# Attention with a mixer on one Trainium2 core: the products with v over 64 columns of TensorE

## The reference, cut to what matters

```python
B, H, S, D = 4, 8, 576, 64
q_rot, k_rot = rotate(q), rotate(k)                       # rotary embedding
scores = q_rot @ k_rot.T / sqrt(D)
attn = exp(scores - max(scores)); attn /= sum(attn) + 1e-9
x = (attn @ v) laid out as [B, S, H * D]
h = max(x.T @ w_tok1, 0) @ w_tok2                         # mixer
u = x + h.T
out = u + max(u @ w_ch1, 0) @ w_ch2
```

## Time and profile before

| | |
|---|---|
| median of 3 runs | 677.58 us (674.8 to 677.66) |
| the profiled execution, its own time | 677.07 us |
| its span, first to last instruction | 675.2 us |
| PE busy in the span | 650.1 us (96%) |
| DVE, ACT, POOL busy in the span | 449.6, 390.2, 296.1 us |
| first V of tile 4, first pair to last pair | 29.67 to 319.92 us |

### The profile page before, as it was taken

How to read it: one execution, slowest core, us unless ns; L and a number is a source line. 1 busy time by engine, 2 the same in 40 slices (tenths; PEclk the granted TensorE clock), 3 DMA queues, 4 the chain that set the end, 5 groups by cost and what they waited for, 6 DMA issues and landing times.

```text
span 675.2 us, 19627 instructions
## 1 busy us (share of the span) xinstructions
PE 650.1 (96%) x7796; PEld 627.6 (93%) x7796; DVE 449.6 (67%) x844; ACT 390.2 (58%) x725; POOL 296.1 (44%) x276
## 2 busy tenths in 40 slices
PE   3999999999999999999999999999999999999997
PEld 2999999999999999999899999999999999999997
DVE  5576766666766666666545598548974489644895
ACT  3455556565555565665547355677646775476753
POOL 4656567766665566522570000484004840048300
PEclk9999999999999999999999999999999999999999
DMA  4234433344433544311600233100031000310002
GB/s 131 73 99 116 130 87 107 101 109 112 116 108 104 149 111 134 87 53 34 205 2 1 63 126 102 48 1 2 2 102 47 0 0 2 99 48 1 1 2 71
DMA packets 52177, 48.73 MB, mean 72 GB/s; under 512 B 15104, under 2 KB 44352, under 8 KB 52096
## 3 DMA queue, kind: packets, MB, share of 16 engines
q1 hardware_dynamic: 51792, 47.52, 24.8%
q10 hardware_dynamic: 304, 0.07, 0.0%
HBM read 30.77 MB, written 9.44 MB: 60 GB/s over the span
## 4 chain that ended last, share of the span: by engine, by line
PE 96%; ACT 1%; DVE 1%; issue 0%; DVEq 0%
PE rest L648 24%; PE slot L604 10%; PE slot L1158 8%; PE slot L1160 8%; PE slot L1159 8%; PE rest L543 7%; PE rest L1158 6%; PE rest L1160 6%; PE rest L1159 6%; PE slot L600 3%; PE slot L1190 2%; PE rest L1190 2%; PE slot L543 1%; PE rest L224 1%; PE rest L221 1%; ACT pt L762 1%
## 5 line engine op out<-in xcount | busy, mean ns | idle before, releaser
L648 PE MATMUL rest<-v,pt 64*128 64x65 f32 x2304 | 152.5, 272 | 7.8 <-ACT pt L762 7.1
L648 PEld LDWEIGHTS rest<-v,pt 64*128 64x128 f32 x2304 | 147.0, 189 | 10.9 <-ACT pt L762 9.4
L840 DVE TENSOR_REDUCE neg_max<-slot 128x1 f32<-128x576 f32 x144 | 108.6, 756 | 71.1 <-PE slot L604 67.8
L1149 POOL TENSOR_TENSOR w_ch_part<-w_ch_sums,w_ch_part 128x512 fp32r<-128x512 f32 x21 | 31.0, 1475 | 178.0 <-ACT w_ch_part L1400 178.0
L762 ACT ACTIVATE pt<-rest 128x320 f32<-128x320 f32 x128 | 55.6, 435 | 88.6 <-PE rest L543 88.6
L1464 ACT ACTIVATE pieces<-h 128x288 fp32r<-128x288 f32 x168 | 73.8, 444 | 49.9 <-PE slot L1160 26.4
L604 PE MATMUL slot<-turned_k,turned_q 64*128 64x288 f32 x256 | 88.2, 436 | 2.3 <-ACT moved_q L776 1.6
L604 PE MATMUL slot<-moved_k,moved_q 64*128 64x288 f32 x256 | 88.2, 436 | 0.0
L1555 DVE TENSOR_TENSOR pieces<-h,pieces 128x288 fp32r<-128x288 f32 x168 | 74.3, 452 | 9.3 <-ACT pieces L1464 8.8
L851 DVE COPY pt<-rest 128x320 f32<-128x320 f32 x128 | 61.7, 482 | 14.8 <-PE rest L543 14.8
L751 ACT ACTIVATE prob_a<-slot,neg_max 128x576 f32<-128x576 f32 x80 | 59.2, 740 | 15.9 <-DVE neg_max L840 12.8
(11 more groups left out here) (248 smaller groups left out, 1922.8 us busy)
## 6 DMA issues: line engine op xcount, KB each, us to landing
moved_q<-turned_q SPq DMA_DIRECT2D x31, 160.0 KB, 2.5
raw_qk<-in_q_dram SPq DMA_DIRECT2D x16, 256.0 KB, 2.6
raw_v<-in_v_dram SPq DMA_DIRECT2D x16, 256.0 KB, 2.7
x_scratch<-x_pair SPq DMA_DIRECT2D x16, 256.0 KB, 2.0
stage_or_x<-x_scratch SPq DMA_DIRECT2D x16, 256.0 KB, 4.0
raw_qk<-in_k_dram SPq DMA_DIRECT2D x15, 256.0 KB, 2.9
w_ch_whole<-in_moe_w_ch_dram SPq DMA_DIRECT2D x8, 384.0 KB, 3.5
w_ch_A_whole<-in_moe_w_ch_dram SPq DMA_DIRECT2D x4, 768.0 KB, 7.8
```

What stands on the lines that cost most here:

```text
L648: return pe.matmul(rest[:, 2 + r, at:at + V], x[rows, j, :], w[rows, j, :], start=begins, stop=ends, skip_group_check=True)
L840: dve.tensor_reduce(neg_max[p % 2][:, i:i + 1], score_slot(p, i)[:, :, 0:HALF], AX.XY, ALU.max, negate=True).then_inc(maxed, 1)
```

## The change

The diff is cut to its core. What it does:

- V no longer splits the 128 rows of the array but its 128 columns. One product contracts all 128 keys of a chunk and has only 64 query columns as weights (`cols`); its output is 64 partitions. The two query halves of a tile are two such products, one for columns 0 to 63 and one for 64 to 127. A tile has 10 products in every case (the tail chunk takes keys 448 to 575, and the rows of `v` that would count twice are zero). Tile 4 takes v of head A for its upper queries and v of head B for its lower ones, so `pt_both` and its zeros go.
- The sum of a head is complete in one bank: head A in bank 2, head B in bank 3. `sum_o` and `y` are gone. `guard` reads the bank, and `normalise` moves from POOL to DVE and reads the bank too.
- V calls stand in groups, (5, 6), (7, 8), (0), (1, 2), (3, 4), and score calls too. There are 7 `pt` buffers in place of 5 and the two `pt_both`.
- The first V of a head waits for that head's `normalise` of the pair before (`x_done`) in place of `o_summed`.
- On SP `store(p - 1)` stands behind `move("k", 0, p + 1)`. The v tail is one transfer and no longer two.

```diff
-    TURNED = 5
+    TURNED = 7
-    RAW = {"k": 2 * 16, "q": 3 * 16, "v": 3 * 16}
+    RAW = {"k": 2 * 16, "q": 3 * 16, "v": 2 * 16}
...
+    def output(h):
+
+        t0, t1 = HEADS[h]
+        return rest[:, 2 + "AB".index(h), 0:(t1 - t0) * V].rearrange("p (t d) -> p t d", d=V)
...
-            store(p - 1)
             if not no(p + 1):
                 sp.wait_ge(scores, p * TILES + G + 1)
             move("k", 0, p + 1)
+            store(p - 1)
             move("q", 0, p + 1)
...
         def values(p, i):
...
-            elif i == 0:
-                pe.wait_ge(o_summed["B"], p)
             if i == 0:
                 pe.wait_ge(v_copied, 2 * p + 1)
             if i == G:
-                pe.wait_ge(o_summed["A"], p + 1)
                 pe.wait_ge(v_copied, 2 * p + 2)
...
+            if p > 0 and i in (0, G):
+                pe.wait_ge(x_done, 2 * (p - 1) + a + 1)
+            to = output("AB"[a])[:, i - HEADS["AB"[a]][0], :]
+            for j in range(NG):
+                for r, cols in enumerate((top, low)):
+                    w = v_sb[r if i == G else a][:, j, :]
+                    mm = pe.matmul(to[cols], pt_of(p, i)[:, j, cols], w, start=(j == 0), stop=(j == G), skip_group_check=True)
             mm.then_inc(o_added, 1)
...
-        def sum_o(p, h):
-            if no(p):
-                return
-            t0, t1 = HEADS[h]
-            dve.wait_ge(o_added, p * TILES + t1)
-            if p > 0:
-                dve.wait_ge(x_done, 2 * (p - 1) + "AB".index(h) + 1)
-            dve.tensor_reduce(y[h][:].rearrange("p t d -> p (t d)"), rest[:, 2:4, 0:(t1 - t0) * V].rearrange("p r n -> p n r"),
-                              AX.X, ALU.add).then_inc(o_summed[h], 1)
...
+        def normalise(p, h):
+            if no(p):
+                return
+            a, (t0, t1) = "AB".index(h), HEADS[h]
+            dve.wait_ge(inv_done, 2 * p + a + 1)
+            if p > 0:
+                dve.wait_ge(x_stored, p * STORED)
+            dve.tensor_tensor(x_pair[:, 1 - a:NG, a, :], output(h)[:, :, 0:D],
+                              inverse[p % 2][:, t0:t1].unsqueeze(2).broadcast_to([P, t1 - t0, D]), ALU.mult).then_inc(x_done, 1)
```

More of the change, by code:

```diff
@@ L536, in gpsimd @@
                 w1.split_lo(pool, p - (N - 2))
-        normalise(N - 1, "B")
     def tensor(pe):
@@ L617, in turn @@
             pe.wait_ge(exped, g + 1)
[L618 to L619 removed]
             for j in range(NG):
+                at = j * P if j < G else S - P
                 for r, rows in enumerate((top, low)):
[L622 to L624 removed]
+                    mm = half_turn(rest[:, r, j * D:(j + 1) * D], prob[i][rows, at:at + P], r)
             mm.then_inc(turned, 1)
@@ L678, in tensor @@
             score(p, 0)
+            score(p, 1)
             turn(p - 1, 7)
+            values(p - 1, 5)
             values(p - 1, 6)
-            score(p, 1)
             turn(p - 1, 8)
+            score(p, 2)
+            score(p, 3)
+            turn(p, 0)
             values(p - 1, 7)
-            score(p, 2)
-            turn(p, 0)
             values(p - 1, 8)
+            turn(p, 1)
             transposes("k", p + 1)
-            turn(p, 1)
+            score(p, 4)
+            turn(p, 2)
             values(p, 0)
-            score(p, 3)
-            turn(p, 2)
-            score(p, 4)
+            score(p, 5)
+            turn(p, 3)
+            score(p, 6)
             values(p, 1)
-            turn(p, 3)
-            score(p, 5)
             values(p, 2)
@@ L698, in tensor @@
             turn(p, 4)
+            score(p, 7)
+            score(p, 8)
+            turn(p, 5)
             values(p, 3)
-            score(p, 6)
-            score(p, 7)
-            turn(p, 5)
             values(p, 4)
-            score(p, 8)
             turn(p, 6)
-            values(p, 5)
         first, p = slot[0], N
         turn(p - 1, 7)
+        values(p - 1, 5)
         values(p - 1, 6)
@@ L729, in slot_left @@
         elif k == 3:
-            pe.wait_ge(o_summed["B"], N)
+            pe.wait_ge(x_done, 2 * N)
     def scalar(act, h1_of_batch_0):
@@ L757, in copy_up @@
                 return
-            to, before = pt_both[0] if i == G else pt_of(p, i), last_on_pt(p, i)
             act.wait_ge(turned, p * TILES + i + 1)
-            if before is not None and before >= 0:
-                act.wait_ge(o_added, before + 1)
-            act.activation(to[:, :, top], rest[:, 0, 0:NG * D].rearrange("p (j n) -> p j n", j=NG), ACT.Copy).then_inc(up_done, 1)
+            pt_free(act, p, i)
+            act.activation(pt_of(p, i)[:, :, top], rest[:, 0, 0:NG * D].rearrange("p (j n) -> p j n", j=NG), ACT.Copy).then_inc(up_done, 1)
         def weights_hi(n):
@@ L778, in scalar @@
         for p in range(N):
-            copy_up(p - 1, 7)
             exponent(p, 0)
+            exponent(p, 1)
             copy_up(p - 1, 8)
@@ L846, in copy_low, with guard @@
                 return
-            to, before = pt_both[1] if i == G else pt_of(p, i), last_on_pt(p, i)
             dve.wait_ge(turned, p * TILES + i + 1)
-            if before is not None and before >= 0:
-                dve.wait_ge(o_added, before + 1)
-            dve.tensor_copy(to[:, :, low], rest[:, 1, 0:NG * D].rearrange("p (j n) -> p j n", j=NG)).then_inc(low_done, 1)
-        def sum_o(p, h):
+            pt_free(dve, p, i)
+            dve.tensor_copy(pt_of(p, i)[:, :, low], rest[:, 1, 0:NG * D].rearrange("p (j n) -> p j n", j=NG)).then_inc(low_done, 1)
+        def guard(p, h):
             if no(p):
@@ L922, in vector @@
         token.split_lo(dve, 0, 3)
-        sum_o(p - 1, "B")
+        guard(p - 1, "B")
+        invert(p - 1, "B")
         token.split_lo(dve, 0, 4)
-        guard(p - 1, "B")
+        normalise(p - 1, "B")
         w1.split_lo(dve, 2)
-        invert(p - 1, "B")
     def last_store(sp):
```

142 lines of the change are left out of this document (46 added, 96 removed).

## The result

| | before | after |
|---|---|---|
| median of 4 runs | 677.48 us (674.8 to 677.66) | 644.73 us (641.5 to 646.36) |
| ratio | | 0.952, 95% interval 0.948 to 0.956 |
| profiled execution, its span | 675.2 us | 639.5 us (time 641.5) |
| TensorE's mean granted clock | 1.00 | 0.997 |

The changed kernel is 4.8% faster, 32.8 us by the medians. 638 us was predicted, with 612 to 664 as the range.

What follows compares the result with a forecast made beforehand. PE bounds the kernel. Per pair 19.36 - 4.5 (V) + 1.5 (switches) - 0.5 - 0.1 (waits, scores) = 15.7 us, 16.8 with the q move; 15 pairs save 38.4 us, last tiles 0.6: 638 us; range 612 to 664.

Steps and rivals of the forecast that it cites:

- The bound: PE's own work sets the pace; V is bound by loading 128 columns of weights, 56 ns an instruction, not by streaming.
- The price of V: V's 180 instructions a pair, loading 64 columns, fall from 56 to 31 ns each: 4.5 us less per pair.
- Rival 3: Column tiles do not load side by side; V stays at 56 ns an instruction, 691 us; chance 0.14.
- rival 4: Load and product of V take turns, about 108 ns an instruction, near 840 us; chance 0.04.
- The switches: PE going to column tiling for V and back costs 0.3 us a group, 1.5 us a pair; bounds 0.75 to 2.0.
- The removed wait and the other engines: PE's wait for `sum_o` goes, 0.5 us a pair; `x_done` costs nothing; DVE, POOL and ACT add nothing.
- rival 2: Small waits of PE for copies, maxima and exponents add 0.5 to 1.5 us a pair, 645 to 661 us; chance 0.16.
- One sign: Sign that the forecast is right: DVE's idle time ahead of the maxima shrinks to a third.
- The move of q: `moved_q`, behind three stores on SP, lands at 16.3 to 17.3 us; PE idles about 1.1 us once a pair.
- Rival 1: The move of q is hidden: 15.7 or 15.0 us a pair, 622 to 611 us; chance 0.11.

Runs made afterwards that it cites:

- Experiment 6: Also `before_33`: the kernel before, with V streaming 33 columns of v in place of 65, half of v left out; 687.52 us, ratio 1.016.
- experiment 8: The kernel before, with V loading only 64 of its 128 query columns, row halves kept, lower 64 queries of each tile left out; 639.91 us, ratio 0.946.
- store_split: Experiment 2: the changed kernel with only the two small tail stores on SP moved behind the move of q; 622.97 us, ratio 0.922.
- experiment 3: Also `nine_groups`: `store_last` with every V call between two turns or scores of its own, nine groups a pair in place of five; 655.33 us, ratio 0.968.
- experiment 4: `store_last` with one tiny product in row halves between the two V calls of three groups; 642.84 us, ratio 0.950.
- store_last: Experiment 1: the changed kernel with all of store(p - 1) on SP moved behind the move of q; 623.43 us, ratio 0.922.
- experiment 9: The kernel before, with each V product split into two of 64 query columns, four 64 by 64 tiles, nothing left out; 655.85 us, ratio 0.969.
- after_33: The changed kernel with V streaming 33 columns in place of 65, half of v left out; 640.38 us, ratio 0.946.

## Why the prediction was right

**The bound.** V was bound by loading, as the prediction read from the distance of loads in the mixer. Experiment 6 showed that V hardly shrinks with the columns streamed, experiment 8 that it does with the columns loaded.

**The price of V.** 31 ns an instruction was taken, 29.5 measured; 180 x 26.5 ns is 4.8 us a pair, 4.5 was forecast. Rival 3 (56 ns) and rival 4 (108 ns) are out. The Trainium skill, TensorE: Matmul & The Clock Gate, section LDWEIGHTS, has the time of a load go by its columns, an estimate of 53 ns for 64; two such loads side by side every 59 ns agree. The Trainium skill, same page, The mechanism, says that a load overlaps a running product only when the row groups differ (in another sentence it also names a background weight buffer). The runs disagree with that "only": column tiles share all rows, each must load 64 columns and stream 65, some 54 ns, and each starts a product every 59 ns, so its load and its streaming overlap.

**The switches.** 0.3 us a group was taken, and the timeline of after shows 0.28. By subtraction, 19.36 - 0.5 - 0.1 - 4.8 = 14.0, and the pairs of `store_split` that do not wait take 15.54, so 0.31 a group. In after and in both kernels with the stores moved, the scores of tiles 7 and 8 take 1.24 us where other pairs of scores take 1.03, because a load waits for ACT's copy of q:

```profile
198.98 0.18 PEld L592 LDWEIGHTS slot<-moved_k,moved_q 64*128 64x128 f32 x1 [0.40 <-ACT turned_q L704]
```

Without these 0.2 us 0.27 a group are left. Added groups cost 0.27 (experiment 3), a single product among V 0.45 (experiment 4). The terms of the prediction add up to 15.76, and it wrote 15.7. V gained 0.3 us more than forecast and the switches cost 0.15 less; against that stand 0.2 us for ACT's copy of q and, in `store_last`, 0.2 us for the landing, for which there was no term. That 15.73 came out is partly luck.

**The removed wait and the other engines.** The 0.5 us for `sum_o` are gone, and `x_done` has not replaced them. ACT's copies hold PE up for 0.9 us once and, ahead of the scores of tiles 7 and 8, for the 0.2 us a pair just named; rival 2, at half a microsecond a pair or more, did not come. One sign was wrong: DVE's idle time ahead of the maxima fell from 71.1 us to 41.4, not to a third, and it cost nothing. The page of after has it in this group:

```profile
L800 DVE TENSOR_REDUCE neg_max<-slot 128x1 f32<-128x576 f32 x144 | 106.5, 755 | 41.4 <-PE slot L592 34.5
```

**The move of q.** Counted from the scores at 186.07, `x_done` came at 12.2 us (12.3 forecast), SP was through with the stores at 13.7 (13.9), `moved_q` landed at 16.3 (16.3 to 17.3), and PE started at 16.5 (16.8). Experiments 1 and 2 show that the order on SP is the cause. Rival 1, the move hidden, is what those two kernels are: 611 to 622 us was its price, 623 came.

**Where the 3.5 us to the profiled run lie.** The term that was mis-sized is the wait for `moved_q`: 15 waits of 1.1 us were forecast, 16.5 us. Measured were 14 with 18.3 us in total, 1.3 each and up to 2.6. The first round of the loop has no store ahead of its move, and there PE does not wait. The waits are 0.7 us where the move landed in 2.5 us, and longer for two reasons: landings of up to 4.5 us, where the earlier trace rows had 2.4 and 3.4, and in three pairs 1.6 to 2.1 us in which SP issued the two small stores, in place of 1.1. So this term is 1.8 us too small. The stretch of low clock adds 1.7 us, which no term held. Together they are the 3.5 us. The pace agrees: 15 x (17.00 - 16.8) is 3 us, and the mixer's first product starts 36.3 us earlier (325.54 to 289.21), of which 15 x 2.35 are 35.2.

**A better kernel.** `store_last` and `store_split` run in 623 us, 54 us below before and 21 us below after; between the two no difference can be told.

## What to carry to other kernels

Where 20 f32 products with short right sides take as long whatever is streamed, look at how many columns the weights have: tiling that contracts more rows with fewer weight columns can be worth its switches if instructions of one tiling stand in groups. Here it was with groups of 20 (`nine_groups`, 3% faster than before) and more so with 40. After a gain on PE, count the path of the next hand-over anew, with every transfer that stands ahead of it in the same issuing queue; a store there costs its issue time, here 0.3 to 0.6 us for one of 256 KB, and for one of 16 KB 0.5 to 0.6 us and at times over 1.4. Gather calls to save switches only as long as none of them was covering a copy. And read a wait of PE from start to start as well as from the view of waits: with overlapping products part of it shows as no idle time.

## What was not expected of the hardware

- Four 64 by 64 tiles go side by side, products and loads both, at 15 ns an instruction by difference (experiment 9).
- Going to the other tiling and back costs 0.28 us around a group between transposes, 0.45 us when it is a single product among V (experiment 4).
- A wait of 2.6 us of an otherwise full PE was followed by 3.5 us at 1.2 GHz, but waits of 2.2 and 2.3 us in the same run were not. In `after_33` the clock was 0.50 from 82.5 to 85.9 us, behind a wait of only 1.5 us. The length of the wait alone does not tell.
- In `before_33` the clock was at 1.2 GHz for 30.8 us although PE was busy for 29.8 of the 31 us ahead of it, with as many loads as the kernel before and half the columns streamed in V. Right ahead of the fall PE waited for 0.7 us, at 312.67; the kernel before has a wait of 0.7 us at the same place (311.62) and held full speed. Whether the shorter products lead to it, and why, was not settled.
- The landing of the same transfer, 160 KB from SBUF to SBUF, took between 2.4 and 4.6 us in one execution, and SP's issue of the two small stores between 1.1 and 2.1 us. What lengthens either was not traced.
